# A unit of one chunk of all four sequences in place of three chunks of two, with the second unit's norms, lengths and masks made during the first unit's substitution

## The reference

```python
def _attn_ref(q, k, v, beta):
    k_n = k / (np.linalg.norm(k, axis=-1, keepdims=True) + 1e-06)
    for t in range(S):
        kt, vt, bt = (k_n[:, :, t], v[:, :, t], beta[:, :, t, None])
        y[:, :, t] = np.einsum('bhd,bhde->bhe', q[:, :, t], state)
        v_old = np.einsum('bhde,bhd->bhe', state, kt)
        state = state + bt[:, :, :, None] * np.einsum('bhd,bhe->bhde', kt, vt - v_old)

def _moe_ref(x, w_gate, w_val, w_out):
    gate = 1.0 / (1.0 + np.exp(-(x @ w_gate)))
    return gate * (x @ w_val) @ w_out

def _moe2_ref(x, w_skip, w_gate, w1, w2):
    do_compute = x @ w_skip > 0                # other tokens pass unchanged
    ...
    for e in range(E):                         # tokens whose largest logit is e
        y[mask] = gate_w[mask, None] * (np.maximum(xc[mask] @ w1[e], 0.0) @ w2[e])
```

## Time and profile before

| | us |
|---|---|
| median of 3 runs (978.76 to 982.52) | 981.93 |
| the profiled execution | 981.73 |
| its span, first to last instruction | 979.7 |
| first dense matmul starts | 67.9 |
| expert loop starts | 785.0 |
| PE busy | 946.7 |
| DVE busy | 450.5 |

### The profile page before, as it was taken

How to read it: one execution, slowest core, us unless ns; L and a number is a source line. 1 busy time by engine, 2 the same in 40 slices (tenths; PEclk the granted TensorE clock), 3 DMA queues, 4 the chain that set the end, 5 groups by cost and what they waited for, 6 DMA issues and landing times.

```text
span 979.7 us, 23053 instructions
## 1 busy us (share of the span) xinstructions
PE 946.7 (97%) x10087; PEld 629.2 (64%) x10087; DVE 450.5 (46%) x1100; ACT 165.1 (17%) x346; POOL 104.6 (11%) x136
## 2 busy tenths in 40 slices
PE   5999999999999999999999999999999999999995
PEld 5965655666565566566556655665555578878874
DVE  7967754766567457536753673212012211211121
ACT  2121211121121131122112111211110021111110
POOL 2010100011010010101010101001001222222221
PEclk9999999999999999999999999999999999999998
DMA  8830004003100400040031000000910115551400
GB/s 351 319 115 2 26 19 146 26 3 116 57 18 2 176 13 1 20 168 2 2 118 71 1 2 34 18 1 18 374 46 0 60 35 195 204 198 50 156 26 28
DMA packets 30299, 78.75 MB, mean 80 GB/s; under 512 B 4072, under 2 KB 20120, under 8 KB 29312
## 3 DMA queue, kind: packets, MB, share of 16 engines
q1 hardware_dynamic: 20112, 61.46, 17.2%
q10 hardware_dynamic: 6912, 9.55, 2.7%
q0 software_dynamic: 3184, 6.39, 2.2%
HBM read 65.34 MB, written 13.00 MB: 80 GB/s over the span
## 4 chain that ended last, share of the span: by engine, by line
PE 93%; DVE 2%; DMA 2%; issue 1%; POOL 1%; SPq 0%; ACT 0%; ACTq 0%; DVEq 0%; POOLq 0%
PE ps L1099 21%; PE ps L1079 19%; PE ps L1088 19%; PE ps L1152 9%; PE ps L1164 9%; PE ps L940 3%; PE ps L982 2%; PE ps L1038 2%; DMA prod<-in_turned_moe_w_out 1%; PE ps L1012 1%; PE ps L954 1%; PE ps L997 1%; PE ps L966 1%; PE ps L1027 1%; PE ps L1044 1%; PE ps L1137 1%
## 5 line engine op out<-in xcount | busy, mean ns | idle before, releaser
L1099 PE MATMUL ps<-wo,prod 128*128 128x393 f32 x576 | 206.1, 503 | 4.8 <-DVE prod L692 4.7
L1079 PE MATMUL ps<-xT,shared 128*128 128x384 f32 x576 | 204.9, 492 | 0.7 <-ACT xT L859 0.7
L1088 PE MATMUL ps<-xT,shared 128*128 128x384 f32 x576 | 204.7, 492 | 0.0
L692 DVE TENSOR_TENSOR prod<-sig,ps 128x384 f32<-128x384 f32 x96 | 52.9, 554 | 233.5 <-PE ps L1088 232.8
L1099 PEld LDWEIGHTS ps<-wo,prod 128*128 128x128 f32 x576 | 104.5, 189 | 76.5 <-DVE prod L692 8.6
L1079 PEld LDWEIGHTS ps<-xT,shared 128*128 128x128 f32 x576 | 106.7, 190 | 70.2 <-issue 0.8
L1088 PEld LDWEIGHTS ps<-xT,shared 128*128 128x128 f32 x576 | 106.9, 190 | 69.8
L1152 PEld LDWEIGHTS ps<-xgT,arena 128*128 128x128 f32 x816 | 93.7, 192 | 5.1 <-ACT xgT L887 0.8
L1152 PE MATMUL ps<-xgT,arena 128*128 128x128 f32 x816 | 94.0, 275 | 0.6 <-ACT xgT L887 0.6
L864 ACT ACTIVATE sig<-ps 128x384 f32<-128x384 f32 x96 | 47.1, 490 | 272.9 <-PE ps L1079 272.9
L1164 PE MATMUL ps<-arena,hT 128*128 128x384 f32 x272 | 90.5, 486 | 0.0
(11 more groups left out here) (171 smaller groups left out, 707.9 us busy)
## 6 DMA issues: line engine op xcount, KB each, us to landing
arena<-in_moe_w SPq DMA_DIRECT2D x16, 1536.0 KB, 10.6
arena<-in_kq SPq DMA_DIRECT2D x7, 1536.0 KB, 8.3
x_scratch<-x ACTq DMA_DIRECT2D x24, 196.5 KB, 4.1
arena<-in_kn SPq DMA_DIRECT2D x8, 576.0 KB, 4.8
shared<-in_v SPq DMA_DIRECT2D x8, 576.0 KB, 9.5
arena<-in_kr SPq DMA_DIRECT2D x8, 576.0 KB, 4.5
out<-x ACTq DMA_DIRECT2D x24, 192.0 KB, 4.2
prod<-in_turned_moe_w_out SPq DMA_DIRECT2D x1, 2304.0 KB, 12.9
```

The source lines that it names most:

```text
L692: nc.vector.tensor_tensor(prod[:, f, :], sig[:, f % 2, :], ps_m[3 - f % 2][:, 0:CT], ALU.mult)\
L1079: last = nc.tensor.matmul(ps_m[f % 2][:, 0:CT], wg[:, a, f * P:(f + 1) * P], xT[:, a, :], start=(a == 0), stop=(a == KT - 1))
L1088: last = nc.tensor.matmul(ps_m[3 - f % 2][:, 0:CT], wv[:, a, f * P:(f + 1) * P], xT[:, a, :], start=(a == 0), stop=(a == KT - 1))
L1099: last = nc.tensor.matmul(ps_m[t][:, 0:XW], prod[:, a, t * P:(t + 1) * P], wo[:, a, :], start=(a == 0), stop=(a == NF - 1))
```

## The change

A unit becomes one chunk (JS = 1) of all four sequences (SEQ = 4): 256 tokens (CT), NS = 16 systems in the 32 lanes, and Q is 12. There is one recurrence step per unit, over twice as many states, and the state is never reset in between (QS = Q). The dense pieces `gate` and `val` become 128x256, the `out` pieces stay, with two groups of 128 tokens in a unit in place of three. The three `gram` events become `gk` (keys) and `gq` (queries), the three `x_turn` parts one event. The masked scores are laid by four ACT copies of 32 partitions each, in place of one ACT copy and one DVE operation. The keys for the norms have a tile of their own (`kn`), the mask factors too (`fac`), `length` two buffers, so that the next unit's can be made before this unit's substitution ends. `kq` is loaded in two DMAs of 48 partitions, without padding rows; the dense weights are loaded earlier; `hT` and `xgT` move into the tile of `prod`, now `work`. In the order, norms, lengths and masks of unit 1 stand inside unit 0's substitution, and `program_order` is rewritten to count in microseconds.

```diff
-JS = 3
-SEQ = 2
+JS = 1
+SEQ = 4
...
+DENSITY = 0.8
+COST = {"gate": 1.29, "val": 1.29, "out": 2.03}
...
+    def substitution(q):
+        return [(("turn_in", q, 0), 2.1)] +             [(("solve", q, u), 0.41 + 0.0021 * u * (H2 - 1 - u)) for u in range(1, H2 - 1)] + [(("from_lanes", q, 0), 5.3)]
+
+    order += [("norm", 0, 0), ("gk", 0, 0), ("lengths", 0, 0), ("mask", 0, 0), ("gq", 0, 0), ("mask", 0, 1)]
+    order += [("turn_in", 0, 0), ("router", 0, 0), ("gk", 1, 0), ("gq", 1, 0), ("warm", 0, 10)]
+    first = [event for event, _ in substitution(0)[1:]]
+    order += first[:12] + [("norm", 1, 0)] + first[12:24] + [("lengths", 1, 0), ("mask", 1, 0), ("mask", 1, 1)] + first[24:]
+    order += [("router_copy", 0, 0), ("off", 0, 0), ("warm", 1, 1), ("pt", 0, 0), ("off", 0, 1), ("warm", 1, 2)]
+    behind += substitution(1)
...
+            if q + 1 < Q:
+                behind.insert(0, (("norm", q + 1, 0), 1.9))
+                dense(6.5)
+                order += [("gk", q + 1, 0), ("gq", q + 1, 0), ("pt", q + 1, 0)]
+                behind[0:0] = [(("lengths", q + 1, 0), 0.9), (("mask", q + 1, 0), 0.7), (("mask", q + 1, 1), 0.7)]
+            while ("from_lanes", q, 0) not in order:
+                if left() > 18.0:
+                    piece()
+                else:
+                    order.append(behind.pop(0)[0])
+            if q + 1 < Q:
+                behind += substitution(q + 1)
+            dense(2.2)
             order.append(("off", q, 0))
-            dense(1.2)
+            dense(1.9)
             order.append(("off", q, 1))
-            dense(1.1)
...
+            for stage in ("read", "apply", "write"):
+                order.append((stage, q, 0))
+                dense(1.6)
...
-    QS = 4
+    QS = Q
...
+                for part in range(4):
+                    block = slice(H2 * part, H2 * (part + 1))
+                    last = nc.scalar.activation(dg[block, 0:NS, :], graw[block, q % 2, :, H2 * (part % 2):H2 * (part % 2 + 1)], ACT.Copy)
+                last.then_inc(dg_ready, 1)
```

More of the change, by code:

```diff
@@ L72, in behind @@
         owed[1] = min(owed[1], 0.0)
-    def dense(n):
-        owed[0] += n
-        while pieces and (owed[0] >= 0.5 or pieces[0][0] in light):
-            heavy = pieces[0][0] not in light
-            order.append(pieces.pop(0))
-            if heavy:
-                owed[0] -= 1
-                behind(0.8)
-    def prepare(q):
-        return [(("lengths", q, 0), 0.45)] + [(("mask", q, i), 0.55) for i in range(3)] + [(("turn_in", q, 0), 1.1)] +             [(("solve", q, u), 0.22 + 0.0011 * u * (H2 - 1 - u)) for u in range(1, H2 - 1)]
@@ L86, in scan @@
-    def scan(q):
-        steps = []
-        for j in range(JS):
-            s = q * JS + j
-            if s % (QS * JS):
-                steps.append(("read", s, j))
-            steps += [("apply", s, j), ("write", s, j)]
-        return steps
-    order += [("norm", 0, 0)] + [("gram", 0, i) for i in range(3)] + [event for event, _ in prepare(0)[0:5]]
-    order += [("router", 0, 0)] + [("gram", 1, i) for i in range(3)] + [("warm", 0, 14)]
-    order += [event for event, _ in prepare(0)[5:]]
@@ L98, in program_order, with piece @@
-    order += [("from_lanes", 0, 0), ("router_copy", 0, 0), ("off", 0, 0), ("warm", 1, 2)] + [("pt", 0, i) for i in range(3)]
-    order += [("off", 0, 1), ("norm", 1, 0), ("warm", 1, 2)]
-    for step in scan(0):
-        if step[0:2] == ("apply", 1):
-            later = prepare(1)
-        order.append(step)
-        if step != scan(0)[-1]:
-            order.append(("warm", 1, 1))
-        behind(0.3)
-    order += [("x_turn", 0, a) for a in range(KT)] + [("pt", 1, i) for i in range(3)]
+    def piece():
+        event = pieces.pop(0)
+        order.append(event)
+        us = COST.get(event[0], 0.0)
+        follow(DENSITY * us)
+        return us
@@ new lines, in dense, with left @@
+    def dense(us):
+        owed[0] += us
+        while pieces[0][0] != "x_turn" and (owed[0] > 0.5 or pieces[0][0] not in COST):
+            owed[0] -= piece()
+    def left():
+        return sum(COST.get(event[0], 0.0) for event in pieces)
+    def substitution(q):
+        return [(("turn_in", q, 0), 2.1)] +             [(("solve", q, u), 0.41 + 0.0021 * u * (H2 - 1 - u)) for u in range(1, H2 - 1)] + [(("from_lanes", q, 0), 5.3)]
+    order += [("norm", 0, 0), ("gk", 0, 0), ("lengths", 0, 0), ("mask", 0, 0), ("gq", 0, 0), ("mask", 0, 1)]
@@ L119, in program_order @@
             order.append(("off", q, 0))
-            dense(1.2)
+            dense(1.9)
             order.append(("off", q, 1))
-            dense(1.1)
-            if follows:
-                order += [("norm", q + 1, 0), ("gram", q + 1, 0), ("gram", q + 1, 1), ("pt", q + 1, 0)]
-                dense(1.0)
-                order += [("gram", q + 1, 2), ("pt", q + 1, 1), ("pt", q + 1, 2)]
-                dense(0.7)
-                later = prepare(q + 1)
-            steps = scan(q)
-            gap = max(0.7, (sum(p[0] not in light for p in pieces) - 4.0) / len(steps))
@@ L131, in program_order @@
-            for step in steps:
-                order.append(step)
-                dense(gap)
-        order += pieces
+            dense(1.9)
+            for stage in ("read", "apply", "write"):
+                order.append((stage, q, 0))
+                dense(1.6)
+        while pieces:
+            piece()
     return order
@@ L309, in program @@
     kq_in = [sem(f"kq_in{i}") for i in range(2)]
[L310 removed]
+    k_first = sem("k_first"); q_first = sem("q_first")
     v_in = [sem(f"v_in{i}") for i in range(2)]
```

335 lines of the change are left out of this document (153 added, 182 removed).

## The result

The changed kernel takes 1003.0 us (median, 1001.67 to 1007.66) beside 980.6 of the kernel before on the same chip: ratio 1.0237, 95% interval 1.0195 to 1.0278. Two repeats on other chips gave 1.0218 (1.0182 to 1.0254) and 1.0198 (1.0181 to 1.0215). So the change makes the kernel slower by 2.0 to 2.4%. The profiled execution took 1002.21, its span is 1000.5, 20.8 more than before. The forecast was 990, so the sign was right and the size was 13 us too small.

A forecast was written before the change was run, and what follows sets the result against it. PE work bounds the kernel, plus a start where PE waits for DVE's first substitution. Start -10.7, PE's dense and attention work +0.1, DVE waits +19.0, end 0: +8.4 on 981.7 gives 990 us, range 974 to 1001 (forecast case alone 984 to 996).

The forecast's parts named there:

- The start: Up to the first dense piece: it would come at 57.2 and not 67.91, -10.7 us, bounds -7 and -12.
- the loads are smaller: Ahead of the first `solve`: 0.4 MB of keys for the norms, not 0.6; first `solve` at 13.9, not 17.54.
- the moved norms don't hide: Rival, unit 0's substitution: the mask waits 2 us for unit 1's scores, start wins only 6; 995 us, chance 0.10.
- the clock falls in the start: Rival, PE idle before `off` 0: clock falls, start's passes take 5.6 more, first pieces 2; 998 us, chance 0.11.
- my walk: Start, step by step from `off` 0 at 43.9 through apply, write and x turn: first dense piece at 57.2.
- The x turn: Attention passes beside the dense pieces: x turn, rank and logits together cost +0.6 us.
- DVE beside dense: Dense stretch: PE's new waits for in-order DVE and the slow clock behind one, +19.0 us, bounds +4 and +30.
- Unit 1's wait: First `out` piece waits for the last product behind `solve` steps and `from_lanes`: +6.6 us, bounds 3.8 and 8.
- The rest of dense: PE's work in the dense stretch: pieces +0.9, gaps +2.4, passes +6.0 and +0.6, fewer breaks -9.8; sum +0.1 us.
- The end: After the last `out`: the gather still waits for the store of the last rows, cost 0, at most 2 us.
- The lower bound on unit 1: Wait at unit 1's first `out`: 3.8 us over the usual gap if DVE never idled in the unit.
- cover holds: Rival, units 2 to 5 and the gaps: small lags vanish as DVE has idle time; 976 us, chance 0.30.

The follow-up runs named there:

- e6: Changed kernel with keys and queries loaded in one DMA of 128 partitions with padding rows, as before the change; 1000.6 us, ratio 1.0194.
- e1: Changed kernel with 24 warm matmuls in place of 10 ahead of the first `off` 0; 1002.9 us, ratio 1.0175.
- e5: Changed kernel with unit 1's norm, lengths and masks put back behind unit 0's substitution; 998.5 us, ratio 1.0176.
- e3: Changed kernel with the x turn's transposes all ahead of its ordinary matmuls, not in turn; 993.4 us, ratio 1.0083.
- a1: The changed kernel itself, unchanged, run again on the chip of e12, e13 and e14; 1003.4 us, ratio 1.0198.
- a0: The changed kernel itself, unchanged, run again on the chip of e5, e6 and e7; 1004.7 us, ratio 1.0218.
- e7: Changed kernel with every second `solve` step of units 1 to 11 left out on DVE, results not true; 1000.3 us, ratio 1.0183.
- e14: Changed kernel with only two more dense pieces ahead of `off` 0 in units 2 to 5; 996.4 us, ratio 1.0130.
- e9: Changed kernel with the edits of e3, e5 and e6 together; 988.0 us, ratio 1.0044.
- e10: e9 with two more dense pieces ahead of `off` 0 in units 2 to 5; 976.3 us, ratio 0.9933.
- e13: Changed kernel with only e12's own edit for unit 1; 1000.9 us, ratio 1.0167.
- e12: e10 with unit 1's `from_lanes` behind the last product, `off` 0 behind two `out` pieces, unit 2's masks behind that; 971.9 us, ratio 0.9879.

## Why the prediction was right in sign and 13 us short

The sum was +8.4 on the profiled execution and the span rose by 20.8. The missing 12.4 lie in these steps. The two in the start and the x turn failed; the walk along DVE's order held.

- **The start, -10.7 forecast, -3.5 measured (7.2 missed).** Two steps of it failed. The first: "the loads are smaller" and the router would start at 15. It started at 20.12, since two DMAs of 48 partitions moved a third of the bytes per microsecond of one with 128 (144 against 411 GB/s); e6 shows it. With the router late the mask waited 4.20, and `off` 0 came at 49.0 and not 43.9. That is the rival "the moved norms don't hide", with a wait of 4.2 where it had 2. The second, the clock: from `off` 0 to the first dense piece it took 15.4 where the walk had 13.3 and kernels at full clock take 12.6 (e1, e5). That is the rival "the clock falls in the start", with 2.8 us where it had 7.6. I had given each a chance of its own and treated them as exclusive, and both came. The clock was to hold behind "3.3 us of nothing", since in the earlier trace rows it fell only after 4.5, and to fall if `dn` came over 1 us late. That step is wrong by itself: here it fell at about 50.2, behind a wait of 3.14 us and when PE had been at work again for 1.2, and in e6, with `dn` 0.6 late, behind 3.97. e6's `off` 0 at 44.53 plus the 12.6 of full clock would be 57.1, the first piece of my walk, so the loads and the clock are all that the start lacked. (The walk's terms add up to 57.7 as written; I took 57.2.)
- **The x turn, inside "+0.6" with rank and logits.** It was priced by passes, 1.25 us for 256 tokens, from rows in which passes of one kind stand together. It takes 1.86: 11 x 0.61 = 6.7 missed, the largest term that I mis-sized in the dense stretch. e3 shows it: sorted, it takes 1.01.
- **DVE beside dense, +19.0 forecast, 15.4 measured.** Unit 1's wait 6.4 over the usual gap (forecast 6.6), the slow `out` pieces behind it 1.6 (2.3), `off` 0 in units 2 to 4 3.7 (4.4), `apply` 1.0 (2.4), the gaps 2.7 (3.3). Walking DVE's queue with the order and the durations of the trace gave each wait its place and nearly its size. What it left out is the clock behind the short ones, which this profile does not show and nine of the twelve traces with these waits do. Unit 1's clock varies too. The whole dense stretch is 733.1 us here, 734.7 in a1 and 735.6 in a0, so the term is 15.4 in one execution and 17 to 18 in others.
- **The rest of dense, +0.1 forecast.** 24.6 - 15.4 - 6.7 = 2.5, so 2.4 missed, in the price of 0.35 us for a break or in the blocks. No run separates these.
- **The end, 0 forecast, -0.3 measured.** The gather waited for the store, as argued.

The late unit's period was forecast at 60 to 61 and is 61.22; without the x turn's order it is 60.36. The lower bound on unit 1 ("3.8 if DVE never idled") was worked out from DVE's amount of work. e7 has 11 us less of it and still waits 5.13: the bound should have come from the length of the block that stands ahead of the product. The rival "cover holds" fell at the same place: DVE's idle time covered nothing, because it lies where DVE waits for an earlier product (0.4 to 0.6 us at a time in unit 1) or, in a late unit, behind the block (4.62 us ahead of one product), and no step of the block can use it. The forecast for DVE's waits is near what came by its mechanism and not by luck; but the 3.6 us that it had too much hide half of the x turn's 6.7 in the sum.

## What to carry to other kernels

When a fixed block of work on an in-order engine comes more often, walk the order at each place where it stands ahead of something that is waited for, and give the matrix engine that much work which needs nothing from the blocked one; one number in the order was worth 7.0 us in the changed kernel (e14) and 11.7 between e9 and e10, half of what the change cost. Before work is moved into the stretch that everything waits for, ask what its own inputs wait for. And price a mixed sequence of matrix instructions from rows with the same mixture, never from a count of passes.

## What the runs showed of the hardware

- **The clock.** It fell behind waits of 1.3 to 1.9 us at `off` 0 (1.34 in e13, 1.66 in a1, 1.91 in e9) for some 5 us, and not in each execution (0.68 in the window of a1, 1.00 in that of the first profile). Behind the gaps of 0.97 us at the late `out` pieces it never fell. That the small `off` matmuls around the wait have a part in it is a guess. The earlier trace rows had led me to fear it only behind gaps of over 4 us. The Trainium skill, page "TensorE: Matmul & The Clock Gate", section "Why this matters for your kernels", warns of idle gaps between bursts; the traces here agree for the 6.9 us gap and show more, a fall behind much shorter ones. Of all kernels only the one before and e12 show 1.00 in every window from 0 to 800 us. In the start the column doesn't tell PE's speed: it reads 1.00 from 20 to 44 us in all traces, yet 128 `gram` passes take 3.75 us there (L921 above) and 2.14 in the earlier trace rows.
- **Loads of part of the partitions.** Two DMAs of 48 partitions each kept the 16 DMA engines 97% busy at 144 GB/s; with one of 128 partitions, a quarter of its rows unused, the same window had 411 GB/s at 101%, and the weights queued behind came 4.5 us earlier.
- **Transposes and products in turn.** The 24 passes of an x turn take 1.86 us when the two kinds alternate, with seven changes of kind, and 1.01 when they are sorted, with one: some 0.14 us for each change, if the changes are what costs.
